# Second block's tiles of 512 tokens with the last 256 tokens multiplied plainly, and its seven weight sets prepared by GpSimd in the first block and loaded from memory

## What is computed

```python
def _moe_ref(x, w_in, w_out):            # first block: 512 -> 2048 -> 512
    h = np.maximum(x @ w_in, 0.0)
    return (h * h @ w_out).astype(np.float32)

def _moe2_ref(x, w1, w2, w3, w_out):     # second block: 512 -> 1024 -> 512
    a = x @ w1
    b = x @ w2
    h = a * b @ w3
    return (h @ w_out).astype(np.float32)
```

## Time and profile before

| | us |
|---|---|
| median of 3 runs (lowest to highest) | 1298.04 (1297.35 to 1300.06) |
| the profiled execution, its own time | 1296.36 |
| its span, first to last instruction | 1294.7 |
| TensorE busy | 1252.2 (97%) |
| VectorE busy | 817.6 (63%) |
| ScalarE busy | 494.9 (38%) |
| GpSimd busy | 43.6 (3%) |

### The profile page before, as it was taken

The page is one execution under the profiler, slowest core; times in us unless marked ns, Lnnn a source line. Parts: engine busy times, 40 slices in busy tenths (PEclk is TensorE's granted clock), DMA queues, the critical chain, the costliest instruction groups (busy, mean ns, idle before and its releaser), DMA issues.

```text
span 1294.7 us, 19823 instructions
## 1 busy us (share of the span) xinstructions
PE 1252.2 (97%) x7321; PEld 1097.9 (85%) x7321; DVE 817.6 (63%) x1482; ACT 494.9 (38%) x937; POOL 43.6 (3%) x52
## 2 busy tenths in 40 slices
PE   8978999999999999999998869999999999999997
PEld 6656888888888888888888769999999999999997
DVE  6666867666666757565545756665756565666753
ACT  6565554544544545544433432121212121221211
POOL 1000000000000000000003030000000000000000
PEclk9989999999999999999999889999999999999999
DMA  8986531121222121211203310101001010101000
GB/s 303 361 295 209 137 132 52 64 91 50 93 68 82 65 97 49 85 63 46 97 18 129 128 49 1 63 3 60 31 31 61 0 61 0 61 0 61 0 32 31
DMA packets 49696, 105.49 MB, mean 81 GB/s; under 512 B 3648, under 2 KB 8768, under 8 KB 49648
## 3 DMA queue, kind: packets, MB, share of 16 engines
q1 hardware_dynamic: 44768, 83.91, 19.4%
q0 software_dynamic: 4880, 20.97, 4.5%
HBM read 68.17 MB, written 36.70 MB: 81 GB/s over the span
## 4 chain that ended last, share of the span: by engine, by line
PE 90%; DMA 3%; DVE 3%; POOL 1%; ACT 1%; issue 1%; SPq 0%; ACTq 0%; DVEq 0%; POOLq 0%
PE ps_y L638 45%; PE ps_h L638 25%; PE ps_t L638 18%; DMA g_scratch<-g_extra 1%; DMA wp_scratch<-stage 1%; DMA g_scratch<-stage 1%; PE ps_h L697 1%; DVE t L1145 1%; PE ps_t L697 1%; POOL stage L594 1%; DVE X_lo L1145 1%; PE ps_t L662 0%; POOL stT L594 0%; DMA raw<-in_moe_w 0%; DMA raw<-in_moe_w_in 0%
## 5 line engine op out<-in xcount | busy, mean ns | idle before, releaser
L906 ACT CAST v_hi<-t 128x512 fp32r<-128x512 f32 (+2 forms) x216 | 129.0, 597 | 489.0 <-DVE t L1145 489.0
L1145 DVE TENSOR_TENSOR v_lo<-t,v_hi 128x512 fp32r<-128x512 f32 (+2 forms) x216 | 143.6, 665 | 147.0 <-ACT v_hi L906 147.0
L638 PE MATMUL ps_y<-v_hi,X_hi 128*128 128x512 f32 (+1 forms) x576 | 220.1, 382 | 5.9 <-DVE stage L1234 3.3
L638 PE MATMUL ps_y<-v_lo,X_hi 128*128 128x512 f32 (+1 forms) x576 | 218.1, 379 | 0.0
L638 PE MATMUL ps_y<-v_hi,X_lo 128*128 128x512 f32 (+1 forms) x576 | 218.1, 379 | 0.0
L1145 DVE TENSOR_TENSOR t<-t 128x242 f32<-128x242 f32 (+2 forms) x288 | 147.5, 533 | 95.2 <-ACT t L992 92.3
L992 ACT ACTIVATE t<-ps_h 128x512 f32<-128x512 f32 (+1 forms) x144 | 82.6, 573 | 146.3 <-PE ps_h L638 145.8
L638 PEld LDWEIGHTS ps_y<-v_hi,X_hi 128*128 128x128 f32 x576 | 109.1, 189 | 26.5 <-issue 3.7
L638 PEld LDWEIGHTS ps_y<-v_hi,X_lo 128*128 128x128 f32 x576 | 108.8, 189 | 20.4
L638 PEld LDWEIGHTS ps_y<-v_lo,X_hi 128*128 128x128 f32 x576 | 109.0, 189 | 19.4
L1145 DVE TENSOR_TENSOR t<-t,ps_t 128x242 f32<-128x242 f32 (+1 forms) x144 | 76.6, 532 | 41.3 <-PE ps_t L638 38.8
(11 more groups left out here) (249 smaller groups left out, 2874.3 us busy)
## 6 DMA issues: line engine op xcount, KB each, us to landing
raw<-g_scratch SPq DMA_DIRECT2D x64, 256.0 KB
raw<-y_scratch SPq DMA_DIRECT2D x9, 968.0 KB, 5.2
raw<-in_moe_w_in SPq DMA_DIRECT2D x32, 256.0 KB
raw<-in_x_T SPq DMA_DIRECT2D x32, 256.0 KB
raw<-in_x_tok SPq DMA_DIRECT2D x32, 256.0 KB
y_scratch<-stage POOLq DMA_DIRECT2D x8, 1024.0 KB, 5.8
out<-stage POOLq DMA_DIRECT2D x8, 968.0 KB, 4.6
g_scratch<-g_extra SPq DMA_DIRECT2D x14, 512.0 KB, 6.6
```

Of the source, the lines that this page charges most:

```text
L638: mm = nc.tensor.matmul(dst, w, m, start=first and n == 0, stop=last and n == 2)
L906: return nc.scalar.copy(dst, src)
L1145: return nc.vector.tensor_tensor(dst, a, b, op)
```

## The change

The second block takes eight tiles of 512 tokens (42 matmuls of 256 columns and 12 of 512 in a chunk) and then the 256 state rows as a tile of their own without the seven-product scheme: `rest_ab` makes a and b with 2 x 4 x 3 = 24 matmuls of 256 columns, `out_chunk` has 12 of 256, eight chunks of each. For this the set S2 is replaced by the plain block A21, loaded in place near the end (`load_A21`).

The weight sets are made by GpSimd alone, behind the stores of tiles 1 to 4 of the first block, one group behind each (`S_weights`): four loads, four sums, and for each of eight kinds (the seven sets and A21) a cast, a subtraction and a store of both parts to `s_scratch`. SP loads the finished parts straight into their places when those are free. `S_sum`, `S_round`, `S_lower` and their waits are gone from GpSimd, ScalarE and VectorE, and the token sets' splitting keeps its slots.

```diff
+            def load_S(g, part, js):
+                for j in js:
+                    sp.dma_start((S_hi, S_lo)[part][g][j].bitcast(F32), s_dram[g, j, part]).then_inc(S_loaded[g], 16)
...
+            sp.wait_ge(S_stored, 16 * 4 * KINDS)
+            load_S(0, 1, range(N_SETS))
+            sp.wait_ge(h_full, KF * NB)
+            load_S(1, 1, range(N_SETS - 1))
+            sp.wait_ge(h_full, KF * SR + 4)
+            load_S(0, 0, range(N_SETS))
+            sp.wait_ge(h_full, KF * SR + 8)
+            load_S(1, 1, [N_SETS - 1])
+            load_S(1, 0, range(N_SETS))
             sp.wait_ge(piece_split, N_RING)
-            load_S(0)
-            load_S(1)
             sp.wait_ge(y_stored, 16)
-            sp.wait_ge(S_split, N_SETS)
-            load_y(y_tiles[0])
+            load_y(y_main[0])
             sp.wait_ge(wp_stored, 16 * 2)
-            sp.wait_ge(S_split, 2 * N_SETS)
-            for k in range(KG):
-                wait_for(sp, wp_split, k - 3)
-                sp.dma_start(raw[:, 4 + k % 4, :], wp_dram[k]).then_inc(wp_loaded[k % 4], 16)
+            for k in range(4):
+                load_wp(k)
+            for j in range(4):
+                sp.wait_ge(y_full, KF * SR + 9 + j)
+                load_S(2, 0, [j])
+                load_S(2, 1, [j])
             sp.wait_ge(y_stored, 16 * NB)
             sp.wait_ge(set_ready, N_SETS)
-            load_y(y_tiles[1])
+            load_y(y_main[1])
+            for k in range(4, KG):
+                sp.wait_ge(wp_split, k - 3)
+                load_wp(k)
...
+            def S_weights(g):
+                A11, A12, A21, A22, S3 = (top_f[:, k] for k in range(5))
...
+                for dst, row, col in ((A11, 0, 0), (A12, 0, 1), (A21, 1, 0), (A22, 1, 1)):
+                    pool.dma_start(dst, A_block(g, row, col)).then_inc(A_loaded, 16)
+                pool.wait_ge(A_loaded, 16 * 4 * (g + 1))
...
+                def split(src, j):
+                    nonlocal n, stores
+                    wait_for(pool, S_stored, 16 * stores)
+                    wait_for(pool, S_step, n)
+                    nc.gpsimd.tensor_copy(top[:, 5], src).then_inc(S_step, 1)
+                    n += 1
+                    total(top[:, 6], src, top[:, 5].bitcast(F32), ALU.subtract)
+                    pool.wait_ge(S_step, n)
+                    pool.dma_start(s_dram[g, j].rearrange("k p n -> p k n"), top[:, 5:7].bitcast(F32)).then_inc(S_stored, 16)
+                    stores += 1
...
+            store_y(0, S)
+            for g in range(4):
+                store_y(g + 1, S)
+                S_weights(g)
+            for t in range(5, NB):
+                store_y(t, S)
+            store_y(SR, NT)
...
+            def rest_ab(m):
...
+                for dst, sets in ((bank[:, 0:NT], (0, 4)), (bank[:, NT:2 * NT], (1, 5))):
+                    for c in range(KM):
```

More of the change, by code:

```diff
@@ L190, in build_program, with A_block @@
                 v_rows + [raw_r[:, k] for k in range(3)]]
[L192 to L207, removed]
+        def A_block(g, row, col):
+            half, kk = g // 2, g % 2
+            c = 2 * col + kk
+            return (moe2_w1, moe2_w2)[row][c * P:(c + 1) * P, half * C:(half + 1) * C]
         st_zero = sem("st_zero")
@@ new lines, in load_y, with load_wp, load_A21 @@
+            def load_y(src, n=TT):
+                sp.dma_start(raw[:, 0:KM, 0:n], src).then_inc(y_loaded, 16)
+            def load_wp(k):
+                sp.dma_start(raw[:, 4 + k % 4, :], wp_dram[k]).then_inc(wp_loaded[k % 4], 16)
+            def load_A21(half):
+                sp.wait_ge(prod_done, N_SETS * (KG * (NB - 1) + 4 * half + 3) + 2)
+                for g in (2 * half, 2 * half + 1):
+                    for part in range(2):
+                        sp.dma_start((S_hi, S_lo)[part][g][1].bitcast(F32),
+                                     s_dram[g, KINDS - 1, part]).then_inc(A21_loaded[half], 16)
@@ L561, in _ @@
+            load_S(3, 1, range(4, N_SETS))
+            with sp.Fori(0, NB - 2) as i:
+                sp.wait_ge(set_ready, i * N_SETS + 2 * N_SETS)
+                load_y(y_main[i + 2])
+            load_A21(0)
+            sp.wait_ge(y_stored, 16 * (NB + 1))
+            sp.wait_ge(set_ready, N_SETS * NB)
+            load_y(y_rest, NT)
+            load_A21(1)
         @block.gpsimd
@@ L856, in second_block @@
                     out_chunk(t, m - 1)
-                if then:
+                if isinstance(t, int) and t == NB - 1:
+                    rest_ab(0)
+                else:
                     ab_chunk(t + 1, 0)
@@ L894, in _ @@
             second_block(0, wp_ready=first_wp_ready)
-            with pe.Fori(0, TILES - 2) as i:
+            with pe.Fori(0, NB - 2) as i:
                 second_block(i + 1)
-            second_block(TILES - 1, then=False)
+            second_block(NB - 1)
+            for m in range(1, KG):
+                rest_ab(m)
+                out_chunk(SR, m - 1, NT)
+            out_chunk(SR, KG - 1, NT)
         @block.scalar
@@ L1072, in ab_chunk @@
                 copy(P1, bank_W[:, 0:HT]).then_inc(P1_copied, 1)
-                if m == KG - 1 and refill:
-                    for j in range(N_SETS):
-                        set_round(t + 1, j)
+                if m == KG - 1:
+                    if isinstance(t, int) and t == NB - 1:
+                        for j in range(2):
+                            rest_round(j)
+                    else:
+                        for j in range(N_SETS):
+                            set_round(t + 1, j)
                 wait_for(act, out_acc, chunk - 1)
@@ L1404, in _ @@
             first_block(7, S, tile7_slot, h_of(SR, NT), sread_slot)
-            def into_second(f):
-                if f == 0:
-                    ab_chunk(0, 0)
-            def first_S(f):
-                if f == 1:
-                    for g, j in S_chunks[0]:
-                        S_lower(g, j)
-            first_block(SR, NT, sread_slot, into_second, first_S)
+            first_block(SR, NT, sread_slot, lambda f: ab_chunk(0, 0) if f == 0 else None, lambda f: None)
             second_block(0)
-            with dve.Fori(0, TILES - 2) as i:
+            with dve.Fori(0, NB - 2) as i:
                 second_block(i + 1)
-            second_block(TILES - 1, last=True)
+            second_block(NB - 1)
+            for m in range(1, KG):
+                rest_chunk(m)
+            drain_out(SR, NT)
 def kernel(**inputs):
```

228 lines of the change are left out of this document (115 added, 113 removed).

## The result

The changed kernel takes 1301.89 us (median of 20 runs, 1298.1 to 1304.82), the kernel before 1298.25 beside it (20 runs, 1296.04 to 1300.06): a ratio of 1.0028, with a 95% interval of 1.0019 to 1.0037. It is slower by 0.3%, where the prediction had 1273. The profiled span is 1297.2 us after 1294.7.

A forecast was written before the change was run, and what follows sets the result against it. TensorE, busy for 97% of the span, was taken as the bound. Seam -12.2, second part -15.8, tail -1.9, clock +2.5 and GpSimd's work +2 gave -25.4: 1271.0 us profiled, 1273 beside the median, range 1264 to 1291.

The forecast's parts named there:

- GpSimd's work in the first block: Main tiles of the first block: GpSimd's weight-set work slows VectorE and costs +2 us in all.
- GpSimd's own time: First block, behind tile stores: 23.2 us of sums, subtractions and casts per group, 63 us with loads and stores.
- a row that is too long: First block, rival: a group takes 94 to 97 us and tile stores queue behind it, 1307 us; chance 0.05.
- The factor 0.61: First block: VectorE loses 61% of the time overlapped by GpSimd's work, so it grows by 9 us a main tile.
- The lag: Dense slots 4 to 9: VectorE's lag grows by at most 5.8 us against slack 4.25, excess 1.6 a tile at most.
- VectorE and GpSimd go one at a time: Main tiles 2 to 5, rival: VectorE needs 86 us in a tile of 71.9, price 57, 1332 us; chance 0.08.
- Clock and seam to y(15)'s end: Seam: without raw loads, sums and splits y(15) ends at 732.5, not 744.74, -12.2 us; clock loss after stops, +2.5.
- the seam's loads are late: Seam, rival: tokens land 6 us later behind 16 weight loads, +6 and 2 of clock, 1281 us; chance 0.14.
- From there to the last matmul: Second block after y(15): 526.9 us instead of 542.7, -15.8, of which 1.2 are the matmuls.
- Tail: After the last matmul: shorter copies and a smaller store take -1.9 us from 7.2.
- Transfers at nothing: First block: GpSimd's 16.8 MB of stores and 4 MB of loads meet a DMA share of 0.21 and cost nothing.
- Loads of groups 2 and 3 in time: Seam: 28 transfers of 256 KB would be done at 751, before chunk 4 needs them at 755.8.

The follow-up runs named there:

- e2: Changed kernel with GpSimd's sums left out and each subtraction replaced by a second cast, loads and stores kept: 1269.01 us, ratio 0.9778 to the kernel before.
- e6: Changed kernel with GpSimd's pieces released after chunks 2, 3, 6, 9, 12, 14, and SP loading tokens and four `wp` blocks before the weight sets: 1265.6 us.
- e7: Kernel before with only the second block's new tile sizes, weight sets still made at the seam, S2 in place of A21: 1291.29 us, ratio 0.9954.
- e3: Changed kernel without GpSimd's weight-set work except one group's loads and one store, SP loading that block everywhere: 1269.12 us, ratio 0.9783 to the kernel before.
- e1: Changed kernel without GpSimd's 80 sums, casts and subtractions, loads and stores kept: 1269.43 us, ratio 0.9786 to the kernel before.
- e8: Changed kernel with GpSimd's eight pieces in each of tiles 1 to 4 released one by one, two chunks apart: 1281.02 us, ratio 0.9876 to the kernel before.
- e9: Changed kernel with GpSimd's pieces released six a tile, after chunks 4 to 9, the dense slots: 1274.49 us, ratio 0.9819 to the kernel before.

## Why the prediction was wrong

**What failed is one term: "GpSimd's work in the first block", +2.** It measured +31.6 (the store of tile 6 at 648.42 against 616.38, less 0.4 that lay ahead). It was built in three steps.
- *GpSimd's own time* was right. A cast took 0.61 us alone and 0.76 in the mean (0.8 taken), a two-input instruction 1.3 alone, up to 2.1 beside VectorE and 1.43 in the mean (1.4), a store 3.8 to land (4.2), a group's work some 59 to 64 us (63). Only the four loads took 12 us (416.68 to 428.74) instead of 6. The rival of a row that is too long did not come.
- *The factor 0.61* was wrong, and it carried the term. It was the lengthening of 1.09 us divided by the slowed instruction's whole 1.78 us. But in those 1.78 us it also did its own 0.69 us of work. What overlapped it was GpSimd's second sum, in the timeline of POOL of the kernel before:

```profile
706.85 1.36 POOL L594 TENSOR_TENSOR raw<-raw 128x512 f32<-128x512 f32 x1
708.29 1.62 POOL L594 TENSOR_TENSOR stage<-raw 128x512 f32<-128x512 f32 x1
```

From 706.98 to the second sum's end at 708.21 are 1.23 us, of which 1.09 were lost: 89%, all but a full stop. In its last 0.47 us the subtraction ran beside the third sum, and there it was the sum that grew (1.62 us instead of 1.27). The row of before bore out the rival, not the forecast. VectorE then grows by 13.5 us in a tile, as measured, where I had 9.
- *The lag*, for which a full stop in the dense slots 4 to 9 gave a bound of +21 (5.25 a tile), went past that bound, to 7.9 a tile. The pieces go on behind those slots, to the cast, subtraction and store that end at about 475.5 in the timeline of POOL, and the longest wait of TensorE in this tile, 2.86 us, ends at 475.12. TensorE's busy time also grows by 1.3 to 3 us in these tiles, with stretches at 1.2 GHz among it, which I had priced for the seam only.

The rival that came was "VectorE and GpSimd go one at a time" (0.08), in its mechanism and place: tiles 2 to 5, `v_lo` as releaser, and a decision point of 6.9 us per tile, against 7.9 measured. Its price of 57 was too high, since it added casts that cost next to nothing (e2) and left VectorE no idle time to give.

**The other terms held in sum, with errors that partly cancel.**
- *Clock and seam to y(15)'s end:* -12.2 + 2.5 forecast. y(15) ends at 768.48, with the last of the 24 matmuls of y(14) and y(15) that start at 765.14. From the eighth store to there it is 54.8 us instead of 62.8, so -8.0 in all against -9.7. The two stops are 1.68 and 3.12 us (1.9 and 2.8 forecast); the 1.66 us ahead of them had not been forecast. Chunk 0 began 2.3 us later than forecast when the 31.7 us are taken off: SP's load was issued at 731.39 as forecast (700.4 + 31.7 = 732.1), but landed 8.3 us after, not 5.2 (the same load before: 5.7). That is the rival "the seam's loads are late" in a mild form; in e6, which issues the load earlier, VectorE no longer waits for it.
- *From there to the last matmul:* 523.1 us instead of 542.7, -19.6 against -15.8. Most of the difference is the second block's tiles: 61.64 us instead of 62.08, since a 256-column matmul in that stream comes every 118 ns (4.95 us / 42, 961.14 to 966.09), where I had 120 from the rest tile's stream. e7 shows the term by itself, with the tail: -6.0, where the sum had -3.1. By the gap of N/2.4 + 2.5 ns in the Trainium skill ("TensorE: Matmul & The Clock Gate", Back-to-back issue gap) the term alone would be an estimated +1.8; e7 doesn't agree.
- *Tail:* 5.6 us instead of 7.2, -1.6 (-1.9).
- *Transfers at nothing:* borne out by e3. *Loads of groups 2 and 3 in time:* yes, no wait for them.

Sum by the trace: +31.7 - 8.0 - 19.6 - 1.6 = +2.5, by which the spans differ. Without the first term the forecast is 1271, and e1, which has no such work, took 1269.4. That it comes so near is in part luck: the seam gave 1.7 us less than forecast and the second block 3.8 more.

What stays open: why some squares are stopped for 1.75 us by a sum of 1.30 us. There are eight in the four tiles, 2.43 to 2.46 us long. All were started while GpSimd issued the store ahead of that sum, 0.5 to 0.6 us before the sum itself, and ended 0.55 to 0.57 us behind it, so a VectorE instruction can be stopped by a sum that starts after it. Nor did any run part sums from subtractions. That e8 loses more than e9 may be by its number of pieces or by the piece at a tile's first chunk; that was not tried.

## What to carry to other kernels

Before work is put on GpSimd beside a VectorE that is 64% busy, add up GpSimd's two-input time over the stretch in which VectorE is densest and set it against the slack of the one result that TensorE waits for, not against the tile's mean. That sum warns but is no price: here it gave 5.25 us a tile where 7.9 were lost, and in e8 a loss of next to nothing where 2.8 were. Take the work as a full stop, and where it must be done, release it piece by piece by VectorE's own progress: here the same 80 instructions cost 32 us back to back and nothing when six a tile were spread. And when a factor of contention is read from one slowed row, divide by the overlap with the other engine's instruction, not by the slowed length.

## What had not been expected of the hardware

- The two engines wait for each other: GpSimd's subtraction took 1.29 us alone and 2.14 when VectorE's 1.22 us instruction was under way, and VectorE's next one then took 1.77 instead of 0.69.
- One-input casts on GpSimd (0.61 us for 128 x 512) lengthened VectorE's tile by 1.4 to 2.6 us for sixteen of them, a tenth of a microsecond or so each; two-input ones of 1.3 us cost 1.13 us each in the mean, those without any VectorE instruction beside them included.
- Four loads of 256 KB on GpSimd's queue, issued right behind the 1 MB store of a tile, were awaited until 12.1 us after the first issue, 9.9 after the last.
